# Another order of the slot work around block 2 of a routed feed-forward kernel on one Trainium2 core

## What is computed

```python
# 1: attention, 4 batches, 8 heads, 576 positions, head size 64
#    heads 0-3: the 32 last positions; heads 4-7: every 32nd position
# 2: tokens x (2304, 512)
h = x @ w_in                                 # (2304, 1024)
solu = h * softmax(h)
x = layernorm(solu) * g_ln @ w_out           # (2304, 512)
# 3: experts
logits = x @ w_gate + modality_bias[modality_id]
e_idx = argmax(logits, axis=1)
gate_w = softmax(logits)[e_idx]
out[t] = gate_w[t] * (relu(x[t] @ w1[e_idx[t]]) @ w2[e_idx[t]])
```

## Time and profile before

| | us |
|---|---|
| median of 3 runs (616.5 to 618.93) | 616.84 |
| the profiled execution | 618.93 |
| its span in the trace | 617.2 |
| PE busy in the span | 593.7 |
| DVE busy | 309.1 |
| ACT busy | 234.0 |
| POOL busy | 146.2 |

### The profile page before, as it was taken

The page is one execution under the profiler, slowest core; times in us unless marked ns, Lnnn a source line. Parts: engine busy times, 40 slices in busy tenths (PEclk is TensorE's granted clock), DMA queues, the critical chain, the costliest instruction groups (busy, mean ns, idle before and its releaser), DMA issues.

```text
span 617.2 us, 11299 instructions
## 1 busy us (share of the span) xinstructions
PE 593.7 (96%) x3655; PEld 490.5 (79%) x3656; DVE 309.1 (50%) x735; ACT 234.0 (38%) x728; POOL 146.2 (24%) x151
## 2 busy tenths in 40 slices
PE   4899999998999999999999999999999999999995
PEld 3666767677888788888888888997998987788894
DVE  5899999865666666656665613436211200021210
ACT  3788888843333334333434322211221211111210
POOL 5455555541001000242224101010011021101001
PEclk9999999998999999999999999999999999999998
DMA  8966776300000070000000000004910026100000
GB/s 177 188 158 163 172 166 161 90 1 19 17 17 32 20 282 26 18 34 17 17 17 34 18 17 17 16 34 152 395 64 17 32 89 253 35 16 32 15 16 34
DMA packets 69035, 47.47 MB, mean 77 GB/s; under 512 B 54840, under 2 KB 56856, under 8 KB 69008
## 3 DMA queue, kind: packets, MB, share of 16 engines
q1 hardware_dynamic: 66928, 41.08, 23.2%
q0 software_dynamic: 2080, 6.03, 2.8%
HBM read 37.66 MB, written 10.22 MB: 78 GB/s over the span
## 4 chain that ended last, share of the span: by engine, by line
PE 77%; issue 9%; POOL 6%; DVE 3%; SPq 2%; DMA 1%; ACT 1%; POOLq 0%; DVEq 0%; ACTq 0%
PE bank L573 16%; PE pair L971 16%; PE pair L573 15%; PE bank L986 15%; POOL work L545 4%; PE pair L1610 3%; PE pair L1620 3%; PE pair L1079 3%; POOL w_lo L552 2%; PE bank L1099 1%; DMA arena<-in_k 1%; SPq L422 1%; PE pair L1111 1%; PE pair L694 1%; PE bank L705 1%
## 5 line engine op out<-in xcount | busy, mean ns | idle before, releaser
L971 PE MATMUL pair<-x_hi,lead_hi 128*128 128x256 f32 x288 | 82.3, 286 | 0.6 <-DVE lead_h L1031 0.6
L971 PE MATMUL pair<-x_hi,lead_lo 128*128 128x256 f32 x288 | 81.5, 283 | 0.0
L971 PE MATMUL pair<-x_lo,lead_hi 128*128 128x256 f32 x288 | 81.5, 283 | 0.0
L765 ACT ACTIVATE work<-pair,neg_max 96x128 f32<-96x128 f32 (+2 forms) x176 | 61.5, 367 | 18.9 <-PE bank L705 15.3
L1520 POOL TENSOR_TENSOR rstd<-ln_small 128x1 f32 (+1 forms) x18 | 26.4, 1466 | 173.0 <-DVE ln_small L640 173.0
L1042 POOL DMA_INDIRECT out<-work,lead_sidx x18 | 18.0, 1001 | 198.8 <-ACT work L1026 167.6
L573 PE MATMUL pair<-w_hi,x_hi 128*128 128x512 f32 x144 | 58.4, 406 | 0.2 <-ACT arena L754 0.2
L573 PE MATMUL bank<-w_hi,lnT_hi 128*128 128x512 f32 x144 | 57.1, 396 | 1.1 <-DVE lnT_lo L1273 1.1
L545 POOL TENSOR_TENSOR work<-work,row_inv 96x512 f32<-96x512 f32 (+3 forms) x48 | 44.7, 931 | 55.3 <-DVE row_inv L853 55.3
L573 PE MATMUL bank<-w_hi,lnT_lo 128*128 128x512 f32 x144 | 56.7, 394 | 0.0
L573 PE MATMUL bank<-w_lo,lnT_hi 128*128 128x512 f32 x144 | 56.6, 393 | 0.0
(11 more groups left out here) (217 smaller groups left out, 1210.4 us busy)
## 6 DMA issues: line engine op xcount, KB each, us to landing
entry<-in_moe_w SPq DMA_DIRECT2D x12, 1024.0 KB, 13.8
arena<-in_q SPq DMA_DIRECT2D x32, 144.0 KB, 2.9
arena<-in_k SPq DMA_DIRECT2D x32, 144.0 KB, 3.4
x_dram<-work SPq DMA_DIRECT2D x18, 256.0 KB, 2.0
arena<-in_moe_w SPq DMA_DIRECT2D x8, 512.0 KB, 7.7
arena<-in_v SPq DMA_DIRECT2D x16, 144.0 KB, 2.5
work<-in_v SPq DMA_DIRECT2D x16, 135.0 KB
arena<-in_moe_w_in SPq DMA_DIRECT2D x8, 256.0 KB, 3.1
```

The lines of the kernel that those rows point to most:

```text
L765: ins = act.activation(probs[g % 2][0:rows, cols], score_ps[g % 2][0:rows, cols], ACT.Exp, bias=neg_max[g % 2][0:rows, n:n + 1], accum_out ...
L971: ins = pe.matmul(lead_h_ps[n % 2][:, jj * BLK:(jj + 1) * BLK], a[:, w], b[:, x], start=(passes == 1), stop=(passes == 3 * KC))
```

## The change

Around block 2 it puts the slot work into another order on DVE and on PE. No operation is added or removed.

```diff
@@ solu_dve @@
             order(dve.scalar_tensor_tensor(out=first_slot[:, :], in0=lead_hot, scalar=FAR, in1=first_slot[:, :],
                                            op0=ALU.mult, op1=ALU.add))
+            place_tokens()
+            build_slots(0)
             lead_rest_h(dve, 2, 0)
-            place_tokens()
             lead_rest_h(dve, 2, 1)
-            build_slots(0)
-            lead_rest_h(dve, 2, 2)
-            lead_rest_h(dve, 2, 3)
-            lead_stage_scatter(dve, 2)
 
             order(dve.tensor_scalar(has, others, 1.0, None, ALU.min))
...
             dve.tensor_copy(meta[:, 2:E + 2], incl).then_inc(meta_ready, 1)
 
             build_slots(1)
+            lead_rest_h(dve, 2, 2)
+            lead_rest_h(dve, 2, 3)
+            lead_stage_scatter(dve, 2)
             lead_rest_x(dve, 3, 0)
             lead_rest_x(dve, 3, 1)
             build_slots(2)
@@ experts_pe @@
-            for n in range(4):
-                lead_up(pe, 2, n)
+            lead_up(pe, 2, 0)
             sum_slots(0)
+            lead_up(pe, 2, 1)
+            lead_up(pe, 2, 2)
+            sum_slots(1)
+            lead_up(pe, 2, 3)
             lead_down(pe, 2, 0)
-            sum_slots(1)
+            sum_slots(2)
             lead_down(pe, 2, 1)
-            sum_slots(2)
```

## The result

The changed kernel is slower. In the first comparison its median was 623.52 us (620.99 to 623.84, 6 executions) against 617.29 us (616.5 to 618.93, 6); the ratio is 1.0088, with a 95% interval of 1.0068 to 1.0108. In a second one on another occasion it was 623.08 against 617.65, ratio 1.0085 (1.0070 to 1.0101). I had forecast +4.43 us and 621.3; measured are +6.2 and +5.4 us. The profiled execution took 621.45 us, its span was 619.7.

What follows compares the result with a forecast made beforehand. PE's queue was taken to bound the kernel, 77% of the chain of waits. Net wait 3.03 plus clock 1.40 gave +4.43 us on the median 616.84: 621.27, stated as 621.3, range 619.5 to 622.8.

Steps and rivals of the forecast that it cites:

- Nothing waits before `sum_slots(0)` or `sum_slots(2)`: PE in block 2: `sum_slots(0)` ready with cover of 2.7 us, `sum_slots(2)` 0.23 us early.
- The wait before `sum_slots(1)`: PE comes at 414.17, DVE's signal at 418.48 after meta chain and build: PE stands still 4.31 us.
- The wait's net price: Wait of 4.31 us in block 2 less the 1.28 us lost before: +3.03 us, bounded by 2.7 and 3.4.
- Rests of quarters 2 and 3 and the scatter's copy late: On DVE behind `build_slots(1)`: later than before, yet ahead of what needs them, so no cost.
- Weights earlier: SP issues the entries' weights from about 419.1, 5 us earlier; first use is at 498.40, so no gain.
- A fall of the clock: PE computes nothing for 3.99 us in block 2, so its clock falls at about 417.87, during the wait.
- the term of the clock: After the fall in block 2, 2.81 us of low clock meet matmuls at half speed: +1.40 us, ends 0 and 1.89.
- the row: Profile of before: clock fell at 142.50 for 3.42 us; 24 matmuls took 7.33 us instead of 5.44, a loss of 1.89.
- rival D: More than one low-clock stretch (array stays low longer), or `sum_slots(2)` waits too: 622.98 us, chance 0.05.
- the rule of the half: Skill's rule: loss is half the throttled time; 1.71 us for the 3.42 us fall, making the sum +4.74.

Runs made afterwards that it cites:

- third trace: The changed kernel timed once more without an edit, for its trace: that execution took 623.95 us, block 2 30.25 us.
- the kernel with a filler: Changed kernel plus 16 unread 128x512 matmuls on PE just ahead of the wait for `sum_slots(1)`: 619.39 us against 617.65 before, ratio 1.0025.
- the version that keeps DVE's order and has no wait: Changed kernel with PE's `sum_slots(1)` back behind `lead_down(2, 0)` and `sum_slots(2)` behind `lead_down(2, 1)`: 616.04 us against 617.65 before, ratio 0.9974.
- run again: The changed kernel without an edit, second comparison: median 623.08 us against 617.65 before; its profiled execution took 622.13 us.
- the fourth: Trace of the changed kernel with 6 and 3 unread matmuls in PE's two gaps near 140 us: median 621.86 us, block 2 31.28 us.
- the filler in the early gaps: 6 and 3 unread matmuls in PE's two gaps near 140 us: kernel before 615.85 us (617.72 without filler), changed kernel 621.86 us.
- the version that has filler and no wait: The version without a wait in block 2, plus 6 and 3 unread matmuls in PE's gaps near 140 us: 614.57 us against 617.23 before, ratio 0.9952.

## Why the prediction was right in direction and short in size

The path and the waits were right in all steps; the behaviour of the clock was not.

- Nothing waits before `sum_slots(0)` or `sum_slots(2)`: so it was.
- The wait before `sum_slots(1)`: forecast 4.31 us, measured 4.23 (and 4.24 in the third trace). Taken apart: the meta chain (3.3 us by moving it away) and the position on PE (2.87 us per quarter).
- The wait's net price was forecast as +3.03; by the kernel with a filler it is +3.25. Most of the 0.2 us are the torn up matmuls: 2.96 and 2.95 us for a quarter that follows a sum, where an unbroken one takes 2.88.
- Rests of quarters 2 and 3 and the scatter's copy late, at no cost: shown by the version that keeps DVE's order and has no wait.
- Weights earlier, at no gain: from 416.49, which is 13.99 us behind the start of block 2, where the forecast of 419.1 was 13.96 behind it. From block 3's start to the end the kernel after took 186.95 us, before 186.57.
- A fall of the clock: forecast, and seen in all five traces with an idle stretch of 2.6 us or more on PE; in the trace with the stretch filled there was none.

What failed is the term of the clock. I priced it at 1.40 us with ends of 0 and 1.89, on the assumption that it "stays low as long as in the row", 3.42 us, from a fall during the wait. Neither case measured is that one. In three traces of the changed kernel (after, run again, third) it fell after the wait's end and stayed low for 3.41 us, at 1.49 to 1.52 us. In the fourth it fell during the wait and stayed low for 6.8 us, at 2.54. That 1.40 comes near 1.49 is luck: I had 2.81 us of low clock meet matmuls and lose half of themselves, where all 3.41 us met them and lost 0.44 of themselves (worked out at the end of this section).

With the filler in the early gaps the long stretch is the common case: five of six executions by their mean clock, and 5.72 - 3.25 = 2.5 us by the mean time. The first half of my rival D, with 0.05 for the whole of it, was this; for that pair it deserved most of the weight. Without that filler the share is known only between bounds. Of the 15 executions of the changed kernel 4 show 0.989, over 13 us at the low level, more than the early fall, one stretch of 3.41 us and the 4.8 at the end can make; in 4 the trace, or a mean clock of 0.996, rules the long stretch out; in the other 7 the mean clock leaves both open. Whether the filler itself shifts the share was not tested.

The row behind the upper end was misread as well. I took the 5.44 us of the next turn for what the 24 matmuls of the earlier trace rows take without a fall. They take 5.72, so that fall cost 1.6 us and not 1.89, and it lies under the 1.71 us by the rule of the half, not above.

The median of the first rounds, 623.52, stands above the top of my range, 622.8; 616.84 times the ratio of 1.0088 is 622.3.

The second error is in the base. I added the difference to a median of three executions without knowing that its executions fall in two groups 1.5 us apart. The median of before lies in the lower one. Of 15 executions of the changed kernel 8 took 623.2 us or more, and the third trace, with both falls, is one of them; so its median can hop by a part of that 1.5 us with no change in the kernel. That it explains the whole step from 5.4 to 6.2 us between the two comparisons was not shown.

By the Trainium skill (TensorE: Matmul & The Clock Gate, section HAM oscillation — how this bites in real kernels) the loss is half of the throttled time. For the stretch of 3.41 us that would be, as an estimate, 1.71 us. The trace and the filler give 1.49. The timeline of PE, kernel after, says why it is less:

```profile
415.83 0.94 PE L1583 MATMUL pair<-slot_col,slot_lo 128*128 128x78 f32 x6 [4.03 <-DVE slot_col L1366]
...
417.57 0.41 PE L971 MATMUL pair<-x_lo,lead_hi 128*128 128x256 f32 x1
417.78 0.41 PE L971 MATMUL pair<-x_hi,lead_lo 128*128 128x256 f32 x1
...
420.26 0.28 PE L971 MATMUL pair<-x_hi,lead_hi 128*128 128x256 f32 x1
420.38 0.28 PE L971 MATMUL pair<-x_lo,lead_hi 128*128 128x256 f32 x1
```

These matmuls of 128x256 start 0.21 us apart at the low level (2.87 / 24 = 0.120 at the high one; over the low stretch, 416.93 to 419.49, the spacing averages 0.213), so that a low microsecond loses (0.213 - 0.120) / 0.213 = 0.44 of itself, and 3.41 times 0.44 is 1.50. The early fall gives the same kind of sum. In PE's timeline of the kernel before its matmuls of 128x512 start 0.43 us apart:

```profile
143.28 0.63 PE L573 MATMUL bank<-w_lo,lnT_hi 128*128 128x512 f32 x1
143.71 0.63 PE L573 MATMUL bank<-w_hi,lnT_lo 128*128 128x512 f32 x1
```

At the high level, in 5.44 us for 24, they are 0.227 apart. The share lost is 0.47, and 3.41 times that is the 1.6 us of the traces.

## What to carry to other kernels

Before an instruction that waits is moved forward on the busiest engine, walk the other engine's queue up to the signal and add what stands in front of it, side work included; here 18 tiny operations, harmless on DVE, became 3.3 us of PE. Count a wait of some us on TensorE twice: once for standing still, and once for matmuls at half clock after it, which lost another 1.5 to 2.5 us here. If the wait must stay, try unread matmuls inside it: 16 of them gave 3.7 us back here, 8 did so only in part of the executions. To price a low stretch, take what the same matmuls cost without it from another execution, and not from their neighbours. And when the executions of a kernel fall in two groups, tell them apart, by the mean clock and by traces, before a difference of 1 or 2 us is believed.

## What had not been expected of the hardware

- The clock can fall after work has begun again: 0.6 us into it in the trace of after, where 4.03 us of idle time lay before. It can also fall 2.9 us into the wait, and then it outlasts 5.7 us of unbroken matmuls.
- Two gaps of PE of 1.39 and 1.06 us, with eight transposes between them, bring a fall in at least 26 of 68 executions, at a price of 1.5 to 1.6 us. With nine unread matmuls in them three kernels show none in their three traces, and none by mean clock and time in the other 21 executions, but for one of 617.02 us at 0.996 that can't be told.
- The last entry's scatter landed in 2.66 to 2.68 us in the traces of all five kernels with unread matmuls and in 3.04 to 3.69 us in the seven traces without them. Here are the two ends, from the chain of the version that has filler and no wait and from that of the kernel after; what links them is open.

```profile
539.61 2.67 DMA out<-xT,s_idx
```

```profile
545.65 3.69 DMA out<-xT,s_idx
```
